# Sparse attention before two expert layers: the first mask and its count as one ScalarE pass, GpSimd's products in another order

## The chip, the cores and the metric

The kernel runs on one core of a Trainium2 chip. The metric is the device time of one launch in microseconds (us). A core has five engines that run their own instruction streams and meet only at semaphores: TensorE (PE in the profile; its weight loads are PEld), VectorE (DVE), ScalarE (ACT), GpSimd (POOL) and SyncE (SP), which here only issues DMAs.

## The reference

Three stages follow one another. Only the first is touched by the change. For each of 32 heads (4 batches by 8 heads) of 576 rows:

```python
scores = scale * np.matmul(q, k.transpose(0, 1, 3, 2))          # 576 x 576 per head
kth = np.partition(scores, -top_k, axis=-1)[..., -top_k:-top_k + 1]   # top_k = 32
mask = scores >= kth
scores = np.where(mask, scores, -1000000000.0)
...
attn = attn / (np.sum(attn, axis=-1, keepdims=True) + 1e-09)
return np.matmul(attn, v)
```

Then the 2304 rows go through a gated layer of 8 experts (each row to one expert, 512 to 1024 to 512) and through a last layer with a softmax-weighted activation and a layer norm.

## The kernel before

`stage_a` does the attention. Two heads make a pair; a pair has NT = 9 tiles of 128 query rows (the ninth holds the last 64 rows of both heads), so there are 16 x 9 = 144 tiles. Everything is float32. Each tile passes through all engines:

- TensorE `scores` (L518) makes the 128 x 576 scores, ScalarE `save_scores` (L306) copies them to SBUF.
- VectorE finds the 24 largest (SURE = 24) from eight chunks of 72: eight MAX8 over the chunks (L425) give 64 candidates, and three MAX8 with two MATCH_REPLACE between them (L453, L458, L461, L464, L470) give the top 24 of those.
- VectorE `work` (L481) marks with 1.0 every score that is below the 24th. GpSimd `rest` (L258) multiplies score by mark, so that what is left is the scores outside the 24. ScalarE `count` (L329) sums the marks, which tells how many scores lie below the 24th.
- VectorE takes the eight largest of the rest (L467), and the pick (L474, a scalar_tensor_tensor of nine elements with a sum) chooses the 32nd value by that count: `thr`.
- VectorE `kept` (L485) marks with 1.0 every score at or over `thr`, and writes over `rests`. GpSimd `mask` (L271) multiplies the exponentials (ScalarE `exp`, L320) by it.
- TensorE turns the result (L526, L527), ScalarE copies it to SBUF (L334, L335), TensorE multiplies by v (L536), ScalarE saves the output (L344).

The order on every engine is written out by hand: one step of VectorE (`quick_step`) handles the last part of tile t, the top 24 of tile t + 1 and the chunks of tile t + 2, interleaved. GpSimd runs rest(t + 1), mask(t), rest(t + 2), mask(t + 1) and so on. The buffers are counted: six for scores (SB), three for probabilities (PB), two for `rests`. A wait is a `wait_ge` on a semaphore; `hold` puts a trivial wait in front of it.

After the 144 tiles `check_quick` takes the minimum of all thresholds. Where a row's count matched none of the nine counts allowed, its `thr` is 0, and a second copy of `stage_a` with the exact method (four MAX8 and three MATCH_REPLACE over all 576 columns) does the whole attention again. In the profiled run it does not.

Of the kernel before, what the change touches and what calls it, by code (L numbers as in the profile page):

```python
# [21 lines left out]
P = 128  # L22
# [21 lines left out]
AHEAD = 4  # L44
RANKED_TOGETHER = (2, 2, 2, 3)
# [16 lines left out]
def at_least(eng, sem, value):  # L62

    if isinstance(value, int) and value <= 0:
        return
    eng.wait_ge(sem, value)

# [10 lines left out]
def build_program(nc, q_t, k_t, v, modality, w_gate, bias, w1, w2, w_in, w_out, g_ln, out):  # L78
    with ExitStack() as ctx:
# [26 lines left out]
        with ExitStack() as ab:  # L106
# [7 lines left out]
            low = sb(ab, "low", [P, PAIRS])  # L114
            again = sb(ab, "again", [1, 1], I32)
            stage_a(nc, q_t, k_t, v, bank, ident, x_all, locals(), True)
            check_quick(nc, bank, ident, low, again)
            stage_a(nc, q_t, k_t, v, bank, ident, x_all, locals(), False)
# [4 lines left out]
def check_quick(nc, bank, ident, low, again):  # L123

    with ExitStack() as ctx:
        row_low = ctx.enter_context(nc.sbuf_tensor("row_low", [P, 1], F32))
        all_low = ctx.enter_context(nc.sbuf_tensor("all_low", [1, 2], F32))
        step, turned = [ctx.enter_context(nc.semaphore(name)) for name in ("check_step", "low_turned")]
        block = ctx.enter_context(nc.Block())

        @block.vector
        def _(dve):
            dve.tensor_reduce(row_low[:, :], low[:, :], AX.X, ALU.min).then_inc(step, 1)
            dve.wait_ge(turned, 1)
            dve.tensor_reduce(all_low[:, 0:1], bank[0][0:1, 0, 0:P], AX.X, ALU.min).then_inc(step, 1)
            dve.wait_ge(step, 2)
            dve.tensor_scalar(all_low[:, 1:2], all_low[:, 0:1], 0.0, None, ALU.is_le).then_inc(step, 1)
            dve.wait_ge(step, 3)
            dve.tensor_copy(again[:, :], all_low[:, 1:2]).then_inc(step, 1)
            dve.wait_ge(step, 4)  # L140

        @block.tensor
        def _(pe):
            pe.wait_ge(step, 1)
            pe.transpose(bank[0][0:1, 0, 0:P], row_low[:, :], ident[:, :]).then_inc(turned, 1)


def stage_a(nc, q_t, k_t, v, bank, ident, x_all, g, quick):
# [3 lines left out]
    const_set = g["const_set"]  # L152
    with ExitStack() as ctx:
        def sem(name):
            return ctx.enter_context(nc.semaphore(name if quick else name + "_again"))

        def sb(name, shape, dt=F32):
            return ctx.enter_context(nc.sbuf_tensor(name if quick else name + "_again", shape, dt))

        def run(eng, program):  # L160

            if quick:
                program()
            else:
                flag = eng.value_load(g["again"][0:1, 0:1], min_val=0, max_val=1)
                with eng.If_ne(eng.to_reg(flag), 0):
                    program()
# [10 lines left out]
        rests = sb("rests", [P, 2, S])  # L178
        unread = sb("unread", [P, S], mybir.dt.bfloat16)
        cand = sb("cand", [P, 2, CAND])  # L180
        below = sb("below", [P, PB])
        pick = sb("pick", [P, TOPK - SURE + 1])
        thr = sb("thr", [P, 2 * NT])
# [9 lines left out]
        max_found = sem("max_found")  # L193
        max_ready = sem("max_ready")
        exped = sem("exped")
        below_ready = sem("below_ready")
        counted = sem("counted")
        rested = sem("rested")
        kept = sem("kept")
        lows = sem("lows")  # L200
# [9 lines left out]
        def _(sp):  # L210
# [11 lines left out]
            def for_later():  # L222

                sp.dma_start(g["mod_sb"][:, :, :], g["modality"]).then_inc(g["route_loaded"], 16)
                sp.dma_start(g["wg_sb"][:, :, :], g["w_gate"].rearrange("(c p) e -> p c e", p=P)).then_inc(g["route_loaded"], 16)
                sp.dma_start(g["wg_heads"][:, :, :], g["w_gate"].rearrange("(h p) e -> p h e", p=DH)).then_inc(g["route_loaded"], 16)
                sp.dma_start(g["bias_sb"][:, :, :].rearrange("p m e -> p (m e)"),
                             g["bias"].rearrange("m e -> (m e)").unsqueeze(0).to_broadcast([P, 2 * E])).then_inc(g["route_loaded"], 16)
                sp.dma_start(g["g_sb"][:, :], g["g_ln"]).then_inc(g["ffn_loaded"], 16)

            def program():
# [7 lines left out]
                if quick:  # L239
                    for_later()  # L240
# [11 lines left out]
        def _(pool):  # L252
            def rest(t, s):

                b = s % PB
                pool.wait_ge(below_ready, t + 1)
                at_least(pool, masked, t - 1)
                pool.tensor_tensor(rests[:, s % 2, :], score[:, s % SB, :], work[:, b, :], ALU.mult).then_inc(rested, 1)  # L258

            def mask(t, s):  # L260
                b = s % PB
                if quick:
                    keeps = rests[:, s % 2, :]
                else:
                    keeps = score[:, s % SB, :]
                    hold(pool, (ranked, t + 1), (exped, t + 1))
                    pool.tensor_scalar(keeps, score[:, s % SB, :], top[:, s % SB, TOPK - 1:TOPK], None,
                                       ALU.is_ge).then_inc(kept, 1)
# [4 lines left out]
            def pair(i, par, more):  # L273
                for j in range(NT):
                    t, s = i * NT + j, par * NT + j
                    if quick and (more or s < 2 * NT - 1):
                        rest(t + 1, (s + 1) % (2 * NT))
                    mask(t, s)

            def program():  # L280
# [3 lines left out]
                if quick:  # L284
                    rest(0, 0)
                (every_pair if quick else all_pairs)(pool, pair)

            if quick:
                pool.memset(x_all[:, :, FULL, :], 0.0).then_inc(const_set, 1)
                pool.memset(ident[:, :], 0.0).then_inc(const_set, 1)  # L290
                pool.wait_ge(const_set, 2)
                pool.affine_select(out=ident[:, :], in_=ident[:, :], compare_op=ALU.not_equal, fill=1.0, base=0,
                                   pattern=[[-1, P]], channel_multiplier=1).then_inc(const_set, 1)

                pool.iota(g["counts"][:, :], pattern=[[1, TOPK - SURE + 1]], base=S - TOPK, channel_multiplier=0,
                          allow_small_or_imprecise_dtypes=True).then_inc(const_set, 1)
                pool.wait_ge(const_set, g["N_CONST"])
# [3 lines left out]
        def _(act):  # L301
# [7 lines left out]
            def negate_max(t, s):  # L309

                j = s % SB
                act.wait_ge(max_found, t + 1)
                act.activation(neg_max[:, j:j + 1], top[:, j, 0:1], ACT.Copy, scale=-SCALE).then_inc(max_ready, 1)

# [7 lines left out]

            def count(t, s):

                b = s % PB
                act.wait_ge(below_ready, t + 1)
                at_least(act, kept, t - PB + 1)
                at_least(act, counted, t)
                act.activation(unread[:, :], work[:, b, :], ACT.Copy, accum_out=below[:, b:b + 1]).then_inc(counted, 1)  # L329
# [21 lines left out]
            def pair(i, par, more):  # L351
                last = par == 1 and not more
                for j in range(NT):
                    t, s = i * NT + j, par * NT + j
                    if quick and (j + 1 < NT or not last):
                        negate_max(t + 1, (s + 1) % (2 * NT))
                    if quick:
                        count(t, s)
# [13 lines left out]
            def program():  # L372
                if quick:
# [1059 lines left out]
```

## Time and profile before

| what | us |
|---|---|
| median of 3 runs (1150.1 to 1154.91) | 1152.74 |
| the profiled execution | 1150.48 |
| its span, from the first to the last instruction | 1148.8 |
| GpSimd's first mask product starts at | 18.36 |
| GpSimd's last but one mask product starts at | 540.54 |
| GpSimd's last mask product starts at | 542.67 |
| the check on the thresholds starts at | 548.49 |

The attention takes 549 us of the 1149. What follows, from 555.7 us on, is routing and the two layers, which the change leaves as they are. In a stage of 144 equal tiles the thing to read is the period: how far one tile's instruction is from the next tile's.

### The profile page before, as it was taken

The page shows a single profiled execution, that of the slowest core. Times are in us where ns is not written, and L with a number is a line of the kernel's source. Part 1 is how long each engine was busy: PE and PEld are TensorE (multiplying, and loading weights), DVE is VectorE, ACT ScalarE, POOL GpSimd, SP SyncE. Part 2 cuts the span into 40 slices and gives each one's busy share as a digit, 9 for nine tenths or more (in the row PEclk, how much of TensorE's full clock was granted, in tenths as well). Part 3 has the DMA queues.
Part 4 walks back from the last instruction along what each step waited for, and adds up shares of the span by engine and source line. Part 5 has one row for each costly group of instructions (what it writes and reads, how often), then busy time and mean ns, then how long its engine had stood idle before and what let it go on. Part 6 is the DMA issues. An engine that isn't in the chain of part 4 may idle for free. (4 is left out here: it accounts for less than half of the span.)

```text
span 1148.8 us, 22766 instructions
## 1 busy us (share of the span) xinstructions
PE 972.8 (85%) x6187; PEld 805.9 (70%) x6187; DVE 795.1 (69%) x3415; ACT 559.3 (49%) x1442; POOL 544.2 (47%) x451
## 2 busy tenths in 40 slices
PE   7888888888887887887664899999999999999985
PEld 4666666666665666666443888898988989888874
DVE  6999999999999999998685352534435254352523
ACT  5888777887777877776221221212212121331211
POOL 4888888888888888887262011111111111441101
PEclk9999999999999999999885999999999999999997
DMA  2001111010111110100623101000000102200000
GB/s 66 28 29 33 33 34 34 12 33 23 34 33 33 34 32 13 31 3 2 232 83 133 52 19 38 10 27 18 18 18 18 37 9 100 91 18 17 21 10 7
DMA packets 38199, 43.66 MB, mean 38 GB/s; under 512 B 24785, under 2 KB 24785, under 8 KB 38098
## 3 DMA queue, kind: packets, MB, share of 16 engines
q1 hardware_dynamic: 34738, 32.06, 8.8%
q0 software_dynamic: 3360, 10.49, 2.8%
q8 instruction: 35, 0.57, 0.2%
q14 instruction: 66, 0.54, 0.2%
HBM read 70.84 MB, written 9.96 MB: 70 GB/s over the span
## 5 line engine op out<-in xcount | busy, mean ns | idle before, releaser
L258 POOL TENSOR_TENSOR rests<-score,work 128x576 f32<-128x576 f32 x144 | 232.7, 1616 | 110.2 <-DVE work L481 110.2
L425 DVE MAX8 cand<-score 128x8 f32<-128x72 f32 x1152 | 214.8, 216 | 9.3 <-ACT score L306 9.1
L536 PE MATMUL bank<-v_sb,prob_t 128*128 128x129 f32 (+1 forms) x1440 | 214.2, 286 | 0.0
L271 POOL TENSOR_TENSOR prob<-prob,rests 128x576 f32<-128x576 f32 x144 | 202.2, 1404 | 0.7 <-DVE rests L485 0.7
L536 PEld LDWEIGHTS bank<-v_sb,prob_t 128*128 128x128 f32 (+1 forms) x1440 | 184.3, 191 | 17.8 <-issue 0.2
L526 PE MATMUL bank<-ident,prob 128*128 128x128 f32 x576 | 95.7, 289 | 103.7 <-POOL prob L271 103.5
L518 PE MATMUL bank<-k_sb,q_sb 64*128 64x288 f32 (+1 forms) x576 | 176.7, 432 | 5.0 <-DMA k_sb<-k_t 4.7
L526 PEld LDWEIGHTS bank<-ident,prob 128*128 128x128 f32 x576 | 61.1, 142 | 168.5 <-POOL prob L271 168.5
L334 ACT ACTIVATE prob_t<-bank 128x512 f32<-128x512 f32 x144 | 86.1, 598 | 108.9 <-PE bank L527 108.8
L518 PEld LDWEIGHTS bank<-k_sb,q_sb 64*128 64x128 f32 (+1 forms) x576 | 100.2, 194 | 26.3 <-issue 6.7
L320 ACT ACTIVATE prob<-score,neg_max 128x576 f32<-128x576 f32 x144 | 110.5, 767 | 0.1
L467 DVE MAX8 top<-rests 128x8 f32<-128x576 f32 x144 | 108.9, 757 | 1.7 <-POOL rests L258 1.6
L1078 POOL TENSOR_SCALAR stat<-stat 128x1 f32<-128x1 f32 x20 | 4.5, 227 | 212.5 <-DVE stat L1233 212.4
L329 ACT ACTIVATE unread<-work 128x576 bf16<-128x576 f32 x144 | 96.9, 673 | 0.0
L306 ACT ACTIVATE score<-bank 128x576 f32<-128x576 f32 x144 | 93.1, 647 | 7.1 <-PE bank L518 6.7
L1310 PE MATMUL bank<-h_t_hi,w_hi 128*128 128x256 f32 x320 | 90.1, 281 | 4.6 <-DVE w_lo L1285 4.6
L1310 PE MATMUL bank<-x_t_hi,w_hi 128*128 128x256 f32 x320 | 91.1, 285 | 1.4 <-DVE x_t_lo L1192 1.4
L1136 ACT ACTIVATE e<-bank,stat 128x1024 f32<-128x1024 f32 x20 | 24.1, 1207 | 136.7 <-DVE stat L1218 136.7
L1310 PE MATMUL bank<-x_t_hi,w_lo 128*128 128x256 f32 x320 | 90.2, 282 | 0.0
L1310 PE MATMUL bank<-h_t_hi,w_lo 128*128 128x256 f32 x320 | 90.1, 281 | 0.0
L1310 PE MATMUL bank<-x_t_lo,w_hi 128*128 128x256 f32 x320 | 90.0, 281 | 0.0
L1310 PE MATMUL bank<-h_t_lo,w_hi 128*128 128x256 f32 x320 | 89.9, 281 | 0.0
(177 smaller groups left out, 2134.3 us busy)
## 6 DMA issues: line engine op xcount, KB each, us to landing
raw<-w SPq DMA_DIRECT2D x22, 2048.0 KB
q_sb<-q_t SPq DMA_DIRECT2D x16, 320.0 KB, 3.0
k_sb<-k_t SPq DMA_DIRECT2D x16, 288.0 KB, 3.2
v_sb<-v SPq DMA_DIRECT2D x32, 128.0 KB, 2.3
x_rows<-x_n SPq DMA_DIRECT2D x16, 256.0 KB
win_sb<-w_in SPq DMA_DIRECT2D x1, 2048.0 KB, 8.2
wout_sb<-w_out SPq DMA_DIRECT2D x1, 2048.0 KB, 13.6
v_sb<-v SPq DMA_DIRECT2D x32, 16.0 KB, 2.1
```

The lines of the kernel that those rows point to most:

```text
L258: pool.tensor_tensor(rests[:, s % 2, :], score[:, s % SB, :], work[:, b, :], ALU.mult).then_inc(rested, 1)
L271: pool.tensor_tensor(prob[:, b, :], prob[:, b, :], keeps, ALU.mult).then_inc(masked, 1)
L306: act.activation(score[:, j, :].rearrange("p (b s) -> p b s", b=2), score_ps[s % 2][:, :, 0:HALF], ACT.Copy).then_inc(saved, 1)
L320: act.activation(prob[:, s % PB, :], score[:, j, :], ACT.Exp, bias=neg_max[:, j:j + 1], scale=SCALE).then_inc(exped, 1)
L329: act.activation(unread[:, :], work[:, b, :], ACT.Copy, accum_out=below[:, b:b + 1]).then_inc(counted, 1)
L334: act.activation(prob_t[:, s % 2, 0:FULL, :], pt_ps[:, 0, :], ACT.Copy)
L425: ins = dve.max(cand[:, s % 2, 8 * c:8 * c + 8], score[:, s % SB, c * CW:(c + 1) * CW])
L467: next_best = mark(dve.max(top[:, s % SB, SURE:TOPK], rests[:, s % 2, :]))
L518: last = pe.matmul(score_ps[s % 2][:, half, 0:HALF], q_sb[par][rows, c * P:(c + 1) * P], k_sb[par][rows, half * HALF:(half + 1) * HALF], s ...
L526: pe.transpose(pt_ps[:, 0, c * P:(c + 1) * P], prob[:, s % PB, c * P:(c + 1) * P], ident[:, :])
L536: last = pe.matmul(out_ps[s % 2], prob_t[0:k, s % 2, c, :], v_sb[par][0:k, c, :], start=(c == 0), stop=(c == KC - 1))
L1310: ins = pe.matmul(dst, lhs[a][:, c, l_at], rhs[b][:, c, r_at], start=(c == 0 and n == 0), stop=(c == chunks - 1 and n == len(parts) - 1))
```

## The change

The diff does these things in the attention (now `attend_quick`; the second, exact copy is `attend_again`):

1. VectorE's `work` pass over 576 columns (L481 before) is gone. In its place VectorE multiplies the 24th value, one number per row, by a constant (`edge`, 128 x 1), and ScalarE computes Sign(edge - score * scale) over the 576 columns: +1 below the 24th value, -1 from it upwards. Its accumulated sum (`balance`) is the number below less the number at or above, so the counts that the pick compares with go in steps of two. The separate `count` pass of ScalarE is gone. GpSimd multiplies score by side: what is at or over the 24th turns negative, what is below stays.
2. The scale is 2^40 (1 - 2^-24) on both sides. VectorE's product is rounded to float32; the 24th value itself counts as at or above if ScalarE's product is not rounded before the subtraction. `check_quick` also looks whether any edge has all mantissa bits set, where this does not hold; six small instructions are in front of its transpose instead of one.
3. GpSimd runs mask(t), rest(t + 2). rest(t + 2) now waits for the pick of tile t + 1 (`picked`).
4. VectorE's step spans four tiles (t, t + 2 and t + 3) and has the pick in its middle. The minimum over a pair's thresholds (L492) is gone.
5. TensorE's order is turn, values, scores (before: scores, turn, values); scores run six tiles ahead. The turned tile has five equal transposes (`prob` is padded with zeros to 640 columns), and ScalarE copies it in one instruction.
6. Most waits are one `wait_ge` instead of `hold`.

The diff, cut to what the text below speaks of:

```diff
@@ check_quick @@
-            dve.tensor_reduce(row_low[:, :], low[:, :], AX.X, ALU.min).then_inc(step, 1)
+            dve.tensor_reduce(row_low[:, :], bounds[:, :, :].rearrange("p b t -> p (b t)"), AX.X, ALU.min).then_inc(step, 1)
+            dve.tensor_scalar(digits[:, :], bounds[:, 1, :].bitcast(I32), MANTISSA, None, ALU.bitwise_and).then_inc(step, 1)
...
+            dve.tensor_scalar(in_range[:, :], row_digits[:, :], float(MANTISSA), None, ALU.is_lt).then_inc(step, 1)
+            dve.wait_ge(step, 5)
+            dve.tensor_tensor(row_fine[:, :], row_low[:, :], in_range[:, :], ALU.mult).then_inc(step, 1)
@@ attend_quick @@
+            def rest(t, s):
+
+
+                pool.wait_ge(sided, t + 1)
+                at_least(pool, masked, t - 1)
+                at_least(pool, picked, t)
+                pool.tensor_tensor(rests[:, s % 2, :], score[:, s % SB, :], side[:, s % 2, :], ALU.mult).then_inc(rested, 1)
...
+            pool.iota(g["counts"][:, :], pattern=[[2, TOPK - SURE + 1]], base=S - 2 * TOPK, channel_multiplier=0,
+                      allow_small_or_imprecise_dtypes=True).then_inc(const_set, 1)
+            pool.wait_ge(const_set, g["N_CONST"])
+            rest(0, 0)
+            rest(1, 1)
+            for t in range(TILES):
+                mask(t, t % WRAP)
+                if t + 2 < TILES:
+                    rest(t + 2, (t + 2) % WRAP)
...
+            def take_sides(t, s):
+
+                act.wait_ge(edge_ready, t + 1)
+                at_least(act, rested, t - 1)
+                at_least(act, picked, t - PB + 1)
+                act.activation(side[:, s % 2, :], score[:, s % SB, :], ACT.Sign, bias=g["edge"][:, t:t + 1],
+                               scale=-EDGE_SCALE, accum_out=balance[:, s % PB:s % PB + 1]).then_inc(sided, 1)
...
+            for t in range(4):
+                save_scores(t, t)
+            for t in range(2):
+                negate_max(t, t)
+                exp(t, t)
+            take_sides(0, 0)
+            save_scores(4, 4)
+            take_sides(1, 1)
+            negate_max(2, 2)
+            for t in range(TILES):
+                if t + 2 < TILES:
+                    take_sides(t + 2, (t + 2) % WRAP)
+                if t + 3 < TILES:
+                    negate_max(t + 3, (t + 3) % WRAP)
+                if t + 2 < TILES:
+                    exp(t + 2, (t + 2) % WRAP)
+                if t >= 2:
+                    save_out(t - 2, (t - 2) % WRAP)
+                if t + 5 < TILES:
+                    save_scores(t + 5, (t + 5) % WRAP)
+                save_turned(t, t % WRAP)
...
+                if rest:
+                    wait_all(dve, (rested, t + 1))
+                    dve.max(top[:, s % SB, SURE:TOPK], rests[:, s % 2, :]).then_inc(rest_found, 1)
...
+                if rest:
+                    wait_all(dve, (rest_found, t + 1), (sided, t + 1))
+                    dve.scalar_tensor_tensor(out=pick[:, :], in0=g["counts"][:, :], scalar=balance[:, s % PB:s % PB + 1],
...
+                if chain:
+                    wait_all(dve, (sure_found, c + 1))
+                    dve.tensor_scalar(g["edge"][:, c:c + 1], top[:, jc, SURE - 1:SURE], EDGE, None, ALU.mult).then_inc(edge_ready, 1)
+                if chunks:
+                    candidates(7).then_inc(cand_done, 1)
+                if rest:
+                    wait_all(dve, (picked, t + 1))
+                    dve.tensor_scalar(rests[:, s % 2, :], score[:, s % SB, :], g["thr"][:, t:t + 1], None, ALU.is_ge).then_inc(kept, 1)
@@ stage_a @@
-                if chain:
-                    hold(dve, (rank_step, sure))
-                    dve.tensor_scalar(work[:, b_next, :], score[:, j, :], top[:, j, SURE - 1:SURE], None,
-                                      ALU.is_lt).then_inc(below_ready, 1)
```

How the order moves on VectorE in the middle of the attention, one step, before (the names are out<-in; `work` is the first mask, `thr` the threshold):

```order
L453 MAX top<-cand 128x8
L425 MAX cand<-score 128x8 x2
L458 MATCH_REPLACE cand<-top,cand 128x64
L425 MAX cand<-score 128x8 x2
L461 MAX top<-cand 128x8
L425 MAX cand<-score 128x8 x2
L464 MATCH_REPLACE cand<-top,cand 128x64
L467 MAX top<-rests 128x8
L470 MAX top<-cand 128x8
L425 MAX cand<-score 128x8
L474 SCALAR_TENSOR_TENSOR pick,thr<-counts,below,top 128x9
L425 MAX cand<-score 128x8
```

Behind it stand L481 and L485, the two passes over 576 columns. And the same step of the change (line numbers are those of the changed kernel; `bounds` holds both thr and edge):

```order
L378 MAX top<-cand 128x8
L373 MAX cand<-score 128x8
L384 MATCH_REPLACE cand<-top,cand 128x64
L373 MAX cand<-score 128x8 x2
L389 MAX top<-rests 128x8
L392 MAX top<-cand 128x8
L395 SCALAR_TENSOR_TENSOR pick,bounds<-counts,balance,top 128x9
L373 MAX cand<-score 128x8
L402 MATCH_REPLACE cand<-top,cand 128x64
L373 MAX cand<-score 128x8 x2
L407 MAX top<-cand 128x8
```

Behind it stand a chunk, the edge (L412, 128x1), the last chunk and the one pass that is left (L417, kept). The pick went from the tenth place to the seventh, and seven instructions and kept now stand behind it.

On GpSimd, in the middle of the attention, before:

```order
L258 TENSOR_TENSOR rests<-score,work 128x576 [waits masked,below_ready]
L271 TENSOR_TENSOR prob<-prob,rests 128x576 [waits exped,kept]
L258 TENSOR_TENSOR rests<-score,work 128x576 [waits masked,below_ready]
L271 TENSOR_TENSOR prob<-prob,rests 128x576 [waits exped,kept]
L258 TENSOR_TENSOR rests<-score,work 128x576 [waits masked,below_ready]
```

And in the change:

```order
L266 TENSOR_TENSOR rests<-score,side 128x576 [waits picked,masked,sided]
L271 TENSOR_TENSOR prob<-prob,rests 128x576 [waits exped,kept]
L266 TENSOR_TENSOR rests<-score,side 128x576 [waits picked,masked,sided]
L271 TENSOR_TENSOR prob<-prob,rests 128x576 [waits exped,kept]
L266 TENSOR_TENSOR rests<-score,side 128x576 [waits picked,masked,sided]
```

The two products still alternate. Before, the rest product waits for VectorE's first mask and the mask product behind it finds its operands ready. Now both wait for VectorE in every tile: mask for kept, rest for the pick of the next tile.

## Rows read from the trace of the kernel before

**Rows 1.** The page, its first line: the span.

```profile
span 1148.8 us, 22766 instructions
```

**Rows 2.** Windows: length; busy of PE, PEld, DVE, ACT, POOL; clock, DMA, GB/s.

```profile
18.36:540.54 522.18, 421.92 (x2672) 323.06 (x2672) 517.16 (x2838) 412.32 (x1145) 423.65 (x286) 1.00 0.09 26
```

**Rows 3.** Timeline of VectorE: start, length, engine, line, operation, tiles, idle before.

```profile
402.81 0.51 DVE L485 TENSOR_SCALAR rests<-score,thr 128x576 f32<-128x576 f32 x1
403.24 0.21 DVE L453 MAX8 top<-cand 128x8 f32<-128x64 f32 x1
403.37 0.35 DVE L425 MAX8 cand<-score 128x8 f32<-128x72 f32 x2
403.64 0.07 DVE L458 MATCH_VALUE_LOAD cand<-top,cand 128x8 f32 x1
...
403.83 0.35 DVE L425 MAX8 cand<-score 128x8 f32<-128x72 f32 x2
...
404.69 0.76 DVE L467 MAX8 top<-rests 128x8 f32<-128x576 f32 x1
405.36 0.21 DVE L470 MAX8 top<-cand 128x8 f32<-128x64 f32 x1
...
405.62 0.36 DVE L474 SCALAR_TENSOR_TENSOR pick<-counts,below,top 128x9 f32<-128x9 f32 x1
405.91 0.08 DVE L474 DVE_READ_ACCUMULATOR pick<-counts,below,top 128x1 f32 x1
...
406.06 0.50 DVE L481 TENSOR_SCALAR work<-score,top 128x576 f32<-128x576 f32 x1
```

**Rows 4.** Timeline of GpSimd: first products, one period, last products.

```profile
13.13 1.40 POOL L258 TENSOR_TENSOR rests<-score,work 128x576 f32<-128x576 f32 x1 [9.46 <-DVE work L481]
...
18.36 1.40 POOL L271 TENSOR_TENSOR prob<-prob,rests 128x576 f32<-128x576 f32 x1
...
402.96 1.62 POOL L258 TENSOR_TENSOR rests<-score,work 128x576 f32<-128x576 f32 x1 [0.68 <-DVE work L481]
404.55 1.40 POOL L271 TENSOR_TENSOR prob<-prob,rests 128x576 f32<-128x576 f32 x1
406.63 1.62 POOL L258 TENSOR_TENSOR rests<-score,work 128x576 f32<-128x576 f32 x1 [0.68 <-DVE work L481]
...
540.54 1.40 POOL L271 TENSOR_TENSOR prob<-prob,rests 128x576 f32<-128x576 f32 x1
542.67 1.40 POOL L271 TENSOR_TENSOR prob<-prob,rests 128x576 f32<-128x576 f32 x1 [0.74 <-DVE rests L485]
```

**Rows 5.** Timeline of VectorE: the first pick, and the last kept.

```profile
15.86 0.23 DVE L474 SCALAR_TENSOR_TENSOR pick<-counts,below,top 128x9 f32<-128x9 f32 x1 [0.20 <-ACT unread L329]
16.01 0.09 DVE L474 DVE_READ_ACCUMULATOR pick<-counts,below,top 128x1 f32 x1
...
542.07 0.52 DVE L485 TENSOR_SCALAR rests<-score,thr 128x576 f32<-128x576 f32 x1
```

**Rows 6.** Line L781 (least, median, most ns), timeline of GpSimd, of VectorE.

```profile
L781 DVE TENSOR_SCALAR wout_sb<-wout_sb,g_sb x8: 473/474/9082, 576.0 to 587.4; 128x512 f32<-128x512 f32 x8
...
576.22 9.02 POOL L950 TENSOR_TENSOR win_lo<-win_sb,win_hi 128x4096 fp32r<-128x4096 f32 x1 [10.37 <-DVE win_hi L779]
...
576.44 9.08 DVE L781 TENSOR_SCALAR wout_sb<-wout_sb,g_sb 128x512 f32<-128x512 f32 x1
```

**Rows 7.** Timeline of GpSimd and VectorE: a 128x1 operation beside a long product.

```profile
1011.25 9.06 POOL L1063 TENSOR_TENSOR w_lo<-raw,w_hi 128x4096 fp32r<-128x4096 f32 x1 [11.92 <-ACT w_hi L1110]
...
1016.15 0.14 DVE L1224 TENSOR_SCALAR stat<-stat 128x1 f32<-128x1 f32 x1
```

**Rows 8.** Timeline of ScalarE: the start of the attention, the first count pass.

```profile
13.36 0.65 ACT L306 ACTIVATE score<-bank 128x576 f32<-128x576 f32 x1 [1.27 <-PE bank L518]
...
14.96 0.67 ACT L329 ACTIVATE unread<-work 128x576 bf16<-128x576 f32 x1
15.54 0.19 ACT L329 ACTIVATION_READ_ACCUMULATOR unread<-work 128x1 f32 x1
```

More of the change, by code:

```diff
@@ L44 @@
 AHEAD = 4
+EDGE_SCALE = 2.0**40 * (1.0 - 2.0**-24)
+EDGE = 2.0**40 * (1.0 - 2.0**-24)
+LEAST = 2.0**-60
+MANTISSA = 2**23 - 1
+TILES = PAIRS * NT
+UNITS = [(2 * c, 2 * c + 1) for c in range(FULL)] + [(2 * FULL,)]
 RANKED_TOGETHER = (2, 2, 2, 3)
@@ L66, in at_least, with wait_all @@
     eng.wait_ge(sem, value)
+def wait_all(eng, *counts):
+    for sem, n in counts:
+        eng.wait_ge(sem, n)
 def hold(eng, *counts):
@@ L137, in _ @@
-            dve.tensor_scalar(all_low[:, 1:2], all_low[:, 0:1], 0.0, None, ALU.is_le).then_inc(step, 1)
-            dve.wait_ge(step, 3)
+            dve.wait_ge(step, 7)
+            dve.tensor_scalar(all_low[:, 1:2], all_low[:, 0:1], LEAST, None, ALU.is_le).then_inc(step, 1)
+            dve.wait_ge(step, 8)
             dve.tensor_copy(again[:, :], all_low[:, 1:2]).then_inc(step, 1)
-            dve.wait_ge(step, 4)
+            dve.wait_ge(step, 9)
         @block.tensor
         def _(pe):
-            pe.wait_ge(step, 1)
@@ L252, in _ @@
         def _(pool):
[L253 to L258, printed above, removed]
             def mask(t, s):
                 b = s % PB
[L262 to L268, printed above, removed]
+                keeps = score[:, s % SB, :]
+                hold(pool, (ranked, t + 1), (exped, t + 1))
+                pool.tensor_scalar(keeps, score[:, s % SB, :], top[:, s % SB, TOPK - 1:TOPK], None,
+                                   ALU.is_ge).then_inc(kept, 1)
                 pool.wait_ge(kept, t + 1)
@@ L275, in pair @@
                     t, s = i * NT + j, par * NT + j
-                    if quick and (more or s < 2 * NT - 1):
-                        rest(t + 1, (s + 1) % (2 * NT))
                     mask(t, s)
@@ L283, in program @@
                 pool.wait_ge(ones_set, 2)
[L284 to L297, printed above, removed]
+                all_pairs(pool, pair)
             run(pool, program)
@@ L321, in exp @@
                                bias=neg_max[:, j:j + 1], scale=SCALE).then_inc(exped, 1)
[L323 to L329, printed above, removed]
             def save_turned(t, s):
@@ L354, in pair @@
                     t, s = i * NT + j, par * NT + j
[L355 to L358, printed above, removed]
                     if j + 1 < NT or not last:
@@ L372, in program @@
             def program():
-                if quick:
-                    act.wait_ge(const_set, g["N_CONST"])
                 for j in range(AHEAD):
                     save_scores(j, j)
-                if quick:
-                    negate_max(0, 0)
                 exp(0, 0)
-                (every_pair if quick else all_pairs)(act, pair)
+                all_pairs(act, pair)
             run(act, program)
@@ L487, in quick_pair @@
-            def quick_pair(i, par, more):
-                at_least(dve, lows, i - 1)
-                for j in range(NT):
-                    left = 2 * NT if more else 2 * NT - (par * NT + j)
-                    quick_step(i * NT + j, par * NT + j, chain=left > 1, more=left > 2)
-                dve.tensor_reduce(g["low"][:, bass.ds(i, 1)], thr[:, par * NT:(par + 1) * NT], AX.X, ALU.min).then_inc(lows, 1)
-            def program():
-                if quick:
-                    dve.wait_ge(const_set, g["N_CONST"])
-                    quick_step(-1, -1, first=True)
-                    every_pair(dve, quick_pair)
-                    dve.wait_ge(lows, PAIRS)
-                else:
-                    all_pairs(dve, ranked_pair)
+            def program():
+                all_pairs(dve, ranked_pair)
@@ L556, in program @@
                     scores(j, j, 0)
-                (every_pair if quick else all_pairs)(pe, pair)
+                all_pairs(pe, pair)
             run(pe, program)
@@ L564, in is_first @@
     return isinstance(t, int) and t < n
-def every_pair(eng, pair):
-    for i in range(PAIRS):
-        pair(i, i % 2, i < PAIRS - 2)
 def all_pairs(eng, pair):
```

321 lines of the change are left out of this document (229 added, 92 removed).

## The prediction, made before the changed kernel ran

> **What bounds the kernel now.** I read the views in this order: the windows by stage, then the timelines of VectorE and GpSimd over one tile, then the durations of single instructions where something else runs beside them.
>
> The profiled execution took 1150.48 us, with a span of 1148.8 [rows 1]. The changed part is the attention. From the first mask product at 18.36 us to the last but one at 540.54 are 142 periods [rows 4], so 522.18 / 142 = 3.68 us on average; in the undisturbed middle a rest product starts at 402.96 and the next at 406.63, a period of 3.67. In that stretch VectorE is busy for 517 of 522 us, GpSimd 424, TensorE 422, ScalarE 412 [rows 2]. VectorE looks like the bound, with no idle time. The timeline says more. The first pick, at 15.86, runs while GpSimd stands still: its accumulator is read 0.15 us after it starts. In the middle the pick starts at 405.62 and the read comes 0.29 later, at 405.91 [rows 3, 5]. What it waits for is on GpSimd: the mask product ran from 404.55 for 1.40, to 405.95 [rows 4]. So VectorE seems busy for 0.14 us of each tile in which the pick only stands behind GpSimd's product. VectorE's own work is 3.67 - 0.14 = 3.53.
>
> This makes the bound a loop over two engines. VectorE's first mask starts (402.39, 3.67 before the row at 406.06), the rest product starts 0.57 later, the mask product 1.59 behind it (404.55), the pick is let go 1.36 later (405.91), the next first mask starts 0.15 later: 0.57 + 1.59 + 1.36 + 0.15 = 3.67. That is the whole period.
>
> Two more things must be read, since both of GpSimd's products share something with VectorE. The rest product takes 1.62 where `kept` runs beside its beginning, and 1.40 at 13.13, before any `kept` was there [rows 4]. And the other way round, with the same kind of instruction as `kept` (tensor_scalar, float32, SBUF to SBUF): L781 takes 474 ns in the usual case of its eight, and the one that started at 576.44, when a GpSimd product had been running from 576.22, took 9082 ns. It ended at 585.52, the product at 585.24 [rows 6]. So whichever of the two begins first has the way, and the other stands still: a held tensor_scalar ends 0.28 us after the product that held it.
>
> **The change part by part.** I follow a new period from the start of mask(t), called M. VectorE's `kept` ended 0.08 before it (542.07 + 0.52 to 542.67, [rows 4, 5]) and its next instruction starts 0.08 before an end of `kept` (402.81 + 0.51 against 403.24 [rows 3]), so at M - 0.16.
>
> From there to the pick: MAX8 of the candidates 0.13, one chunk 0.14, match 0.19 (403.64 to 403.83), two chunks 0.27, MAX8 over the rest 0.67 (404.69 to 405.36), MAX8 0.13 [rows 3]. Sum 1.53, so the pick would start at M + 1.37. Two of these now stand nearer to what they need than before: the match is one chunk behind its MAX8, and the pick is 0.80 behind the start of a MAX8 that takes 0.76. Waits can add 0 to 0.10 in all; no row shows them at such a distance, and I take 0.03: M + 1.40. GpSimd's mask product ends at M + 1.40 and is out of the way just then, so the pick is not held: 0.15 to its read, 0.09 for the read [rows 5], 0.08 for GpSimd to see it. Rest(t + 2) starts at M + 1.72. No `kept` runs beside it now, so I take 1.40 and not 1.62: it ends at M + 3.12.
>
> Meanwhile VectorE goes on from the read of the pick at M + 1.55: a chunk 0.15, match 0.19, two chunks 0.27, MAX8 0.13, chunk 0.14, edge, chunk 0.14. The edge is a 128 x 1 operation that the attention did not have before; the nearest row is L1224 with 0.14 in all [rows 7], and as a step to the next 0.08 to 0.14. Sum 1.10 to 1.16, so `kept` is reached at M + 2.65 to 2.71. This is 0.4 before rest(t + 2) ends. By [rows 6] it is held and ends 0.28 + 0.04 (576 columns, not 512) behind it, at M + 3.44, and mask(t + 1) starts at M + 3.52.
>
> **The new period is 3.52**, 0.15 less than 3.67. The ends: no waits at all, 3.49, and a few hundredths of rounding under it, 3.46; waits of 0.10, 3.59. VectorE alone would need 0.43 + 1.53 + 0.03 + 0.15 + 1.10 = 3.24: the pass taken away (0.42 us a tile: its 0.50 less the 0.08 by which the next one starts ahead of its end) and the pick's 0.14 are nearly all gained on VectorE, and GpSimd's chain of two waits takes back two thirds of that.
>
> The Trainium skill states this on the page "SBUF — State Buffer", section "Who interferes with whom": VectorE in a two-port mode and GpSimd take a shared pair of ports as a lock, the one that issues first has it for the whole instruction and the other "fully blocks". The trace agrees, with 9082 ns against 474 in rows 6.
>
> Other engines. ScalarE loses a count pass and one of two copies and gets the sign pass, which I cost as the count pass: 0.67, and its sum at 0.77 [rows 8]. Busy 412 / 142 = 2.90 a tile before [rows 2], so it fits in 3.52. Its deadline: the edge of t + 2 is ready about M - 0.7, the side then at M + 0.3 even if it stands behind a copy, and rest(t + 2) asks for it at M + 1.72. More than a microsecond is left. If that cover went, each tenth would count 14 us. TensorE: 422 / 142 = 2.97 a tile, cover 0.5. The turned tile of t leaves TensorE before the next mask product ends either way; the new order of TensorE and its run six tiles ahead I cost at nothing, hidden in that half microsecond; with the cover gone (period under 3.0) TensorE would be next. The two DMA waits of SyncE only change their place by tiles that are far apart.
>
> The start. Before, mask(0) starts at 18.36. Now ScalarE does four score copies, exp(0) and exp(1) before the first sign pass. The fourth copy starts at 13.36 and ends at 14.01, two small ones and two exps follow (0.67 each as steps, 0.3 for the small ones), so the sign pass starts at 15.65 and its sum is there at 16.42. Rest(0) 16.50 to 17.90, MAX8 over it from 18.00, the pick at 18.86, read at 19.10, rest(1) 19.18 to 20.58, `kept` held to 20.90, mask(0) at 20.98: +2.6.
>
> The end. From the last mask product to the check nothing changes. The last interval, 2.13, has no rest product in it before or after and stays at 2.1. The check gets five more small VectorE instructions and a reduce over 288 numbers instead of 16: 5 x 0.14 (the size of L1224 [rows 7]) to 0.21, and 0.3, with their waits 1.2 us. The sixteen small reduces L492 are inside the old average.
>
> **Sum.** Mask(142) starts at 20.98 + 142 x 3.52 = 520.8, where it was 540.54: -19.7. The check gives +1.2: -18.5. The profiled execution would be 1150.48 - 18.5 = 1132.0. The median of the runs shown is 1152.74, 2.3 above the profiled one, so in its terms 1134.2.
>
> **Rivals.**
>
> *The edge is held too (slower).* If the 128 x 1 edge takes the same way as `kept`, VectorE comes to it at M + 2.43, while the rest product runs, and stands until that is over, at about M + 2.93 (0.19 before its recorded end, as L781's 9082 - 474 ns imply); then edge, chunk and a whole `kept` follow one after the other behind it: 0.08 + 0.14 + 0.51 + 0.08 and the edge's own start, M + 3.75. 142 x 0.23 = 33 more, 1167 us. It decides from a hold of about 0.1 on. Against it: L1224, a 128 x 1 tensor_scalar, took 0.14 at 1016.15 with a GpSimd product running from 1011.25 to 1020.31 [rows 7]. I give it 6 in 100. The same section of the Trainium skill names tensor_scalar among the operations that can take the pair and exempts no size; by that rule alone the edge would be held and this rival would be the forecast. Row 1016.15 speaks against that reading.
>
> *The rest product takes 1.62 whatever runs beside it (slower).* Then 3.74 a period, 142 x 0.22 = 31 more, 1165 us. For it: all steady ones take 1.62. Against it: the one at 13.13 takes 1.40. 4 in 100.
>
> *The redo runs.* If ScalarE rounds the product before it subtracts, the 24th value gives 0 and not -1, no count matches, and the exact copy runs: 144 tiles x 7 passes x 0.67 = 675 us more, about 1810. Nothing in the trace shows such a pass. 2 in 100. The Trainium skill, page "ScalarE: Activation LUTs", section "Step-by-step: what each stage is for", says that scale and bias are one fused multiply-add with a single rounding; no row here shows it.
>
> *`kept` is not held.* If the pass can run beside the rest product, VectorE is the bound with 3.24: 142 x 0.28 = 40 less, 1094 us. Rows 6 are against it. 7 in 100.
>
> *The gain is eaten by waits.* A period of 3.62 to 3.70, from semaphore waits that I take as 0.03 and that add up over the four engines: 1148 to 1160. For it: the new loop crosses between the engines four times, the old one twice. 13 in 100.
>
> **How the numbers follow.** Forecast with its own bounds (3.46 to 3.59, 1126 to 1144): 64 in 100. What is left, 4 in 100, lies under 1126 without `kept` being free. A measurement of this kernel can tell about 0.5%, 5.8 us. Faster: 64 + 7 + 4 = 75 and 2 of the fifth rival's 13, 77. Same: the rest of it, 11. Slower: 6 + 4 + 2 = 12. The range must leave out at most 2 in 10: I take 1120 to 1158, which leaves out the slower ones (12) and the free `kept` (7).
>
> **What would show it.** In the changed kernel's trace: `kept` with a mean near 0.8 us and not 0.51, its end 0.3 us behind a rest product's end; the pick at 0.23, not 0.36; both GpSimd products at 1.40; GpSimd's idle time divided into 0.3 before rest (released by the pick) and 0.4 before mask (released by `kept`); 3.52 from mask to mask. I am wrong if `kept` takes 0.51 with a product beside it, if the edge takes more than 0.2, if the rest product's wait ends on ScalarE's `side`, or if ScalarE or TensorE show no idle time.

## The result, and the profile after

The changed kernel takes 1137.8 us (median of 4 runs, 1136.92 to 1138.4), against 1152.43 for the kernel before (4 runs). The ratio is 0.9872, with a 95% interval of 0.985 to 0.9894: faster by 14.6 us, or 1.3%, with the slowest of its runs 11.7 us under the fastest of the kernel before. The times here and below are medians of the usual executions; one of the six of e3 took 4580.92 us at a granted clock of 0.202 and is left out. The profiled execution took 1136.92 us, where that of before took 1150.48. It is the forecast case, inside its own bounds (1126 to 1144), 3.6 us over the predicted 1134.2.

One tile on GpSimd in the changed kernel, as in [rows 4] (start, length, engine, line, operation, tiles, and in brackets the idle time before with what ended it):

```profile
20.65 1.40 POOL L271 TENSOR_TENSOR prob<-prob,rests 128x576 f32<-128x576 f32 x1 [0.39 <-DVE rests L417]
...
401.82 1.41 POOL L271 TENSOR_TENSOR prob<-prob,rests 128x576 f32<-128x576 f32 x1 [0.40 <-DVE rests L417]
403.58 1.41 POOL L266 TENSOR_TENSOR rests<-score,side 128x576 f32<-128x576 f32 x1 [0.35 <-DVE pick L395]
405.39 1.41 POOL L271 TENSOR_TENSOR prob<-prob,rests 128x576 f32<-128x576 f32 x1 [0.40 <-DVE rests L417]
...
526.07 1.39 POOL L271 TENSOR_TENSOR prob<-prob,rests 128x576 f32<-128x576 f32 x1
```

Both products take 1.41, where the rest product took 1.62. But GpSimd stops twice per tile now, 0.35 us for the pick and 0.40 for kept; before it stopped once, for 0.68. The period is 405.39 - 401.82 = 3.57, and over all 142 it is (526.07 - 20.65) / 142 = 3.56, where it was 3.68.

One thing said ahead of the prediction must be set right, since the argument leans on it. The products themselves stand in the same order in both kernels: rest(0), rest(1), mask(0), rest(2), mask(1) and so on. What is new on GpSimd is only what they wait for, above all the pick of tile t + 1 ahead of rest(t + 2).

The same stretch on VectorE, the rows that answer to [rows 3]:

```profile
403.18 0.22 DVE L395 SCALAR_TENSOR_TENSOR pick<-counts,balance,top 128x9 f32<-128x9 f32 x1
403.33 0.08 DVE L395 DVE_READ_ACCUMULATOR pick<-counts,balance,top 128x1 f32 x1
...
404.20 0.14 DVE L412 TENSOR_SCALAR bounds<-top 128x1 f32<-128x1 f32 x1
404.25 0.23 DVE L373 MAX8 cand<-score 128x8 f32<-128x72 f32 x1
404.40 0.91 DVE L417 TENSOR_SCALAR rests<-score,bounds 128x576 f32<-128x576 f32 x1
405.23 0.21 DVE L378 MAX8 top<-cand 128x8 f32<-128x64 f32 x1
```

The pick is free, 0.22 us instead of 0.36. (Counted in the two orders shown ahead of the prediction, it went from the fourteenth instruction of the step to the eighth, with eight instructions and `kept` behind it; the tenth, seventh and seven given there are miscounted.) The edge runs in the middle of a rest product and takes 0.14. `kept` starts at 404.40 and takes 0.91, where it took 0.51 before, and ends at 405.31, which is 0.32 after the rest product ends (403.58 + 1.41 = 404.99). VectorE shows no idle time at all. Its busy time hides 0.4 us of standing per tile.

The window from the first to the last but one mask product, as [rows 2] (length; busy of PE, PEld, DVE, ACT, POOL; clock):

```profile
20.65:526.07 505.42, 420.48 (x2671) 322.23 (x2672) 504.02 (x2816) 418.80 (x1001) 399.57 (x284) 1.00 0.10 27
```

### The profile page after: what moved, and what is told of

The parts are those of the page before. It is cut to its first block and busy times, and to the rows that moved or that the text cites. A ratio compares the mean times of both kernels' runs of the same rounds, so it can differ in the third digit from the quotient of the medians.

```text
span 1135.2 us, 21099 instructions
## 1 busy us (share of the span) xinstructions
PE 971.1 (86%) x6187; PEld 805.2 (71%) x6187; DVE 783.7 (69%) x3404; ACT 566.6 (50%) x1298; POOL 519.8 (46%) x452
## 5 line engine op out<-in xcount | busy, mean ns | idle before, releaser
L373 DVE MAX8 cand<-score 128x8 f32<-128x72 f32 x1152 | 227.8, 223 | 8.3 <-ACT score L297 8.3
L266 POOL TENSOR_TENSOR rests<-score,side 128x576 f32<-128x576 f32 x144 | 203.0, 1410 | 63.7 <-DVE pick L395 51.2
L445 PE MATMUL bank<-ident,prob 128*128 128x128 f32 x720 | 111.3, 286 | 90.8 <-POOL prob L271 90.8
L445 PEld LDWEIGHTS bank<-ident,prob 128*128 128x128 f32 x720 | 77.0, 142 | 155.1 <-POOL prob L271 154.6
L322 ACT ACTIVATE prob_t<-bank 128x640 f32<-128x640 f32 x144 | 101.2, 703 | 85.1 <-PE bank L445 85.0
L417 DVE TENSOR_SCALAR rests<-score,bounds 128x576 f32<-128x576 f32 x144 | 130.6, 907 | 0.1
L305 ACT ACTIVATE side<-score,bounds 128x576 f32<-128x576 f32 x144 | 110.4, 766 | 2.2 <-DVE bounds L412 2.2
```

The lines of the kernel that those rows point to most:

```text
L305: act.activation(side[:, s % 2, :], score[:, s % SB, :], ACT.Sign, bias=g["edge"][:, t:t + 1], scale=-EDGE_SCALE, accum_out=balance[:, s % ...
L322: act.activation(prob_t[:, s % 2, :, :].rearrange("p c q -> p (c q)"), turned_ps[:, 0:QW], ACT.Copy).then_inc(turned_sb, 1)
L373: ins = dve.max(cand[:, sa % 2, 8 * n:8 * n + 8], score[:, sa % SB, n * CW:(n + 1) * CW])
L417: dve.tensor_scalar(rests[:, s % 2, :], score[:, s % SB, :], g["thr"][:, t:t + 1], None, ALU.is_ge).then_inc(kept, 1)
L445: ins = pe.transpose(turned_ps[:, c * P:(c + 1) * P], prob[:, s % PB, c * P:(c + 1) * P], ident[:, :])
```

## The experiments

The theory is the prediction's: the period is a loop, mask product, pick, rest product, held `kept`, mask product. All experiments start from the changed kernel (1137.8 us). "The period" is always the distance between two mask products, and its mean over 142 tiles is read from the start of the first to the start of the last but one. The rivals are VectorE's total work, TensorE's order, and that `kept` is slow by itself. No run takes single parts out of the change, so how the 0.12 us a tile that it gained divide between the removed pass, the moved pick and the shorter waits is not shown.

### Without the wait for the pick

```diff
             def rest(t, s):
...
                 at_least(pool, masked, t - 1)
-                at_least(pool, picked, t)
```

> Edit: the changed kernel, but rest(t + 2) on GpSimd no longer waits for the pick of tile t + 1. Theory (the period is the loop mask, pick, rest, kept, with the pick just reaching VectorE 0.04 us before the mask product ends and so getting in ahead of the rest product): GpSimd's 0.35 us of idle time before rest falls to about 0.05, the rest product ends 0.29 us earlier, the held kept with it, period 3.57 to about 3.28, 142 tiles x 0.29 = 40 us less, 1097. Rival (the wait is what protects the pick: without it the rest product begins first and holds the pick for its whole length): pick of 1.5 us, period near 4.4, about 1260. Rival (VectorE's own work or TensorE is the bound): 1138.

Measured: 1110.55 us, 27.3 less. GpSimd and VectorE:

```profile
403.43 1.41 POOL L270 TENSOR_TENSOR prob<-prob,rests 128x576 f32<-128x576 f32 x1 [0.40 <-DVE rests L416]
404.98 1.41 POOL L265 TENSOR_TENSOR rests<-score,side 128x576 f32<-128x576 f32 x1
406.79 1.41 POOL L270 TENSOR_TENSOR prob<-prob,rests 128x576 f32<-128x576 f32 x1 [0.39 <-DVE rests L416]
...
404.80 0.22 DVE L394 SCALAR_TENSOR_TENSOR pick<-counts,balance,top 128x9 f32<-128x9 f32 x1
...
406.01 0.70 DVE L416 TENSOR_SCALAR rests<-score,bounds 128x576 f32<-128x576 f32 x1
```

The pick, at 404.80, still gets in before the rest product at 404.98. `kept` is reached at the same distance from the mask product as before (2.58 us) and is held 0.2 us less, since the rest product ends 0.21 earlier. So the wait for the pick cost 3.56 - 3.36 = 0.20 us a tile, not the 0.29 that I had put down: the rest product also waits for the mask product's own semaphore, and behind that it starts 0.14 after the mask product's end (403.43 + 1.41 to 404.98) and not 0.05. VectorE's instructions were not touched, and neither of the two rivals, 1260 and 1138, fits.

### The pick earlier, and later

In e2 two chunks move from ahead of the pick to behind it, in e3 one moves the other way. VectorE executes the same instructions in all three.

```diff
@@ e2 @@
-                if chunks:
-                    candidates(1, 2)
                 if rest:
                     wait_all(dve, (rested, t + 1))
...
                 if chunks:
-                    candidates(3)
+                    candidates(1, 2, 3)
@@ e3 @@
+                if chunks:
+                    candidates(3)
                 if rest:
                     wait_all(dve, (rest_found, t + 1), (sided, t + 1))
...
-                if chunks:
-                    candidates(3)
```

> Edit: the changed kernel, with the two chunk MAX8 that stand ahead of the MAX8 over the rest moved behind the pick. VectorE's work is the same, only the pick comes 0.27 us earlier. Theory: the pick is then held by the mask product until that ends, its read comes 0.05 us before the end (0.16 us earlier than now), so the period goes from 3.57 to 3.41, 142 x 0.16 = 22 us less, 1115, and pick takes 0.35 us again. Rival (VectorE's total work sets the period): 1138 or more, since the hold of the pick is added.

> Edit: the changed kernel, with one chunk MAX8 that stands behind the pick moved ahead of it, so the pick comes 0.13 us later. VectorE's work is the same. Theory (loop through the pick): rest starts 0.13 later, period 3.57 to 3.70, 142 x 0.13 = 19 us more, 1157. Rival (VectorE's total work sets the period, the order does not matter): 1138.

Measured: 1118.64 us for the early pick (19.2 less), 1156.17 for the late one (18.4 more). GpSimd in e2, then in e3:

```profile
403.38 1.40 POOL L271 TENSOR_TENSOR prob<-prob,rests 128x576 f32<-128x576 f32 x1 [0.40 <-DVE rests L415]
404.98 1.41 POOL L266 TENSOR_TENSOR rests<-score,side 128x576 f32<-128x576 f32 x1 [0.20 <-DVE pick L393]
406.79 1.40 POOL L271 TENSOR_TENSOR prob<-prob,rests 128x576 f32<-128x576 f32 x1 [0.40 <-DVE rests L415]
```

```profile
404.23 1.40 POOL L271 TENSOR_TENSOR prob<-prob,rests 128x576 f32<-128x576 f32 x1 [0.40 <-DVE rests L417]
406.12 1.41 POOL L266 TENSOR_TENSOR rests<-score,side 128x576 f32<-128x576 f32 x1 [0.48 <-DVE pick L397]
407.92 1.40 POOL L271 TENSOR_TENSOR prob<-prob,rests 128x576 f32<-128x576 f32 x1 [0.40 <-DVE rests L417]
```

Only the bracket before the rest product moves: 0.20, 0.35, 0.48. The periods are 3.41 and 3.69 (3.42 and 3.68 as means). In e2 the pick takes 0.34 again, because it is now there before the mask product ends. One chunk of 0.13 us more in front of the pick costs 18.4 us, more than the whole gain of the change, with the same instructions on VectorE: its total work is not the bound.

### Is `kept` held, or slow by itself?

```diff
-                    dve.tensor_scalar(rests[:, s % 2, :], score[:, s % SB, :], g["thr"][:, t:t + 1], None, ALU.is_ge).then_inc(kept, 1)
+                    dve.tensor_scalar(rests[:, s % 2, :], score[:, s % SB, :], g["thr"][:, t:t + 1], 0.0, ALU.is_ge, ALU.add,
+                                      accum_out=n_kept[:, :]).then_inc(kept, 1)
```

> Edit: the changed kernel, with kept also writing out a sum that nobody reads, which makes it another form of tensor_scalar. Theory (kept takes 0.91 us because the rest product holds it, and this form is not held): it takes 0.6 to 0.75 us beside the running product, with 0.08 for the sum, mask starts 3.45 to 3.55 us after the mask before, 1121 to 1135. Rival (kept takes 0.91 for another reason, or every form is held): 0.91 and more, plus the read of the sum, period 3.65, 1149 or more.

Measured: 1123.79 us, 14.0 less. Two rows of GpSimd and two of VectorE from the middle, then the last `kept` of the attention and the mask product behind it:

```profile
403.19 1.42 POOL L267 TENSOR_TENSOR rests<-score,side 128x576 f32<-128x576 f32 x1 [0.36 <-DVE pick L396]
404.89 1.41 POOL L272 TENSOR_TENSOR prob<-prob,rests 128x576 f32<-128x576 f32 x1 [0.28 <-DVE rests L418]
...
404.00 0.80 DVE L418 TENSOR_SCALAR_CACHE_REDUCE rests<-score,bounds 128x576 f32<-128x576 f32 x1
404.73 0.08 DVE L418 DVE_READ_ACCUMULATOR rests<-score,bounds 128x1 f32 x1
...
512.69 0.81 DVE L418 TENSOR_SCALAR_CACHE_REDUCE rests<-score,bounds 128x576 f32<-128x576 f32 x1
...
513.59 1.41 POOL L272 TENSOR_TENSOR prob<-prob,rests 128x576 f32<-128x576 f32 x1 [0.97 <-DVE rests L418]
```

This form is slower alone, 0.81 us at 512.69 while GpSimd stands idle for 0.97, against some 0.50 for the plain form. But it is not held: in the middle it takes 0.80, from 404.00 to 404.80, while the rest product runs to 404.61, and the mask product starts at 404.89. (I had expected 0.6 to 0.75.) In the changed kernel `kept` ended 0.32 after the rest product, here 0.19, and could be earlier if it were reached earlier. That the slower instruction gives the faster kernel shows that the 0.91 us are a hold. The period, 3.45, is now VectorE's own chain: VectorE has no idle time and none of its instructions is held.

The Trainium skill says the same on the page "SBUF — State Buffer", section "Who interferes with whom": the form of tensor_scalar that also writes out its accumulator is excepted from those that can take the shared pair. The trace agrees, with 0.80 us beside a product and 0.81 without one, against 0.91 for the plain form held.

### TensorE's order

The diff puts TensorE's order of before (scores five tiles ahead, first in the step) back; the five equal transposes and the single copy stay.

```diff
-            for t in range(6):
+            for t in range(5):
                 scores(t, t)
             for t in range(TILES):
+                if t + 5 < TILES:
+                    scores(t + 5, (t + 5) % WRAP)
                 turn(t, t % WRAP)
                 if t >= 1:
                     values(t - 1, (t - 1) % WRAP)
-                if t + 6 < TILES:
-                    scores(t + 6, (t + 6) % WRAP)
```

> Edit: the changed kernel, with TensorE's order of before (scores first, five tiles ahead; then turn, values). Theory: TensorE has over 0.5 us of idle time in each period and is not in the loop: 1138, within 3 us. Rival (part of the gain is TensorE's new order): some of the 14.6 us are lost, 1141 to 1152.

Measured: 1138.47 us, period 3.56. The new order of TensorE is worth nothing that can be measured here, and it costs nothing.

### Who asks first

With e1's edit the rest product still waits for the mask product's own semaphore. Three buffers for `rests` instead of two take this wait away.

```diff
-        rests = sb("rests", [P, 2, S])
+        rests = sb("rests", [P, 3, S])
...
-                at_least(pool, masked, t - 1)
-                at_least(pool, picked, t)
+                at_least(pool, masked, t - 2)
```

(and `s % 3` for `s % 2` where `rests` is used.)

> Edit: as e1_no_pick_wait, with three buffers for rests, so the rest product waits for an older mask product and can follow the one before it at once. Theory (the loop is now GpSimd's alone: 1.41 + 0.14 + 1.41 + 0.40 = 3.36): if the pick, which comes 0.04 us before the mask product ends, still gets in first, the 0.14 goes down to 0 or 0.05, period 3.22 to 3.27, 1110 less 13 to 20 = 1090 to 1098. If the rest product now gets in first, the pick is held for the whole product (1.5 us instead of 0.22), period about 4.4, near 1260. The trace says which; VectorE's own work (3.2) allows no less than about 3.22.

Measured: 1251.02 us, 113 more. The trace says which, GpSimd first, then VectorE:

```profile
400.67 1.40 POOL L270 TENSOR_TENSOR prob<-prob,rests 128x576 f32<-128x576 f32 x1 [1.60 <-DVE rests L416]
402.03 1.41 POOL L265 TENSOR_TENSOR rests<-score,side 128x576 f32<-128x576 f32 x1
405.03 1.40 POOL L270 TENSOR_TENSOR prob<-prob,rests 128x576 f32<-128x576 f32 x1 [1.60 <-DVE rests L416]
...
402.03 1.43 DVE L394 SCALAR_TENSOR_TENSOR pick<-counts,balance,top 128x9 f32<-128x9 f32 x1
...
404.45 0.50 DVE L416 TENSOR_SCALAR rests<-score,bounds 128x576 f32<-128x576 f32 x1
```

Both start at 402.03, and the rest product wins. An operation on nine elements stands for 1.43 us (the median of its 144; only at the two ends of the attention is it shorter), and the period is 4.36 here and 4.35 in the mean. TensorE's granted clock is lower in this run, 0.87 between 100 and 500 us where the changed kernel has 1.00, but GpSimd waits for nothing but `kept` in that stretch, and VectorE has no idle time, so this is not what makes the period long. So the changed kernel's wait for the pick does have a purpose when nothing else separates the two products; it is only dearer than needed.

> Edit: as e5_three_rests, with the pick 0.27 us earlier as in e2_pick_early, so it is queued well before the mask product ends. If the one that asks first has the way: the pick is let in at the mask product's end (0.34 us long), the rest product right behind, period 3.25 to 3.35 (VectorE has 0.12 of hold on top of 3.22), 1092 to 1106. If two products of GpSimd back to back keep VectorE out: pick of 1.7 us or more, period about 4.4, near 1260.

This adds e2's diff to e5's. Measured: 1098.56 us. The two products follow each other as closely as in e5, but the pick is ready before:

```profile
401.06 1.42 POOL L270 TENSOR_TENSOR prob<-prob,rests 128x576 f32<-128x576 f32 x1 [0.50 <-DVE rests L414]
402.42 1.43 POOL L265 TENSOR_TENSOR rests<-score,side 128x576 f32<-128x576 f32 x1
...
402.15 0.35 DVE L392 SCALAR_TENSOR_TENSOR pick<-counts,balance,top 128x9 f32<-128x9 f32 x1
```

The same pick is let in when it comes 0.27 us earlier: 1251 against 1099 us, from the place of two MAX8. So it is not that two products back to back keep VectorE out. `kept` takes 0.49 us and is not held any more; VectorE is the bound, with 3.28, of which 0.13 are the pick standing behind the mask product.

> Edit: the changed kernel with both e1's edit (no wait for the pick) and e2's (pick earlier). Theory: the rest product waits for the mask product's own semaphore, 0.14 us, in which the queued pick gets in; VectorE is not the bound, so it is the same as e1_no_pick_wait: period 3.36, 1110. Rival (each of the two edits has its own gain and they add): 1110 - 19 = 1091.

Measured: 1108.87 us, period 3.36, the same as e1 (3.36) within 2 us. The gains of e1 and e2 do not add, since both shorten the same gap before the rest product, down to 0.14.

> Edit: as e6_early_three_rests, with one of the two chunk MAX8 put back ahead of the pick. Theory: what decides is who asks first. The pick is then ready 1.22 us after the mask product starts, the rest product asks at 1.36, so the pick still gets in, and it no longer stands 0.13 us behind the mask product. VectorE's period 3.27 goes to about 3.15; GpSimd's own 1.36 + 1.42 + 0.40 = 3.18 takes over: 3.18 to 3.22, 1098.6 less 7 to 13, 1086 to 1092. Rival (0.14 us is too near and the rest product gets in first): pick of 1.5 us, near 1250, or some tiles so and others not, between.

The diff against e6: `candidates(1)` ahead of the MAX8 over the rest, `candidates(2, 3)` behind the pick. Measured: 1084.83 us, a ratio to the kernel before of 0.9416 (0.9395 to 0.9437). The pick takes 0.22, and the period is 3.18:

```profile
402.65 1.41 POOL L270 TENSOR_TENSOR prob<-prob,rests 128x576 f32<-128x576 f32 x1 [0.40 <-DVE rests L416]
404.02 1.42 POOL L265 TENSOR_TENSOR rests<-score,side 128x576 f32<-128x576 f32 x1
405.83 1.41 POOL L270 TENSOR_TENSOR prob<-prob,rests 128x576 f32<-128x576 f32 x1 [0.39 <-DVE rests L416]
...
403.88 0.22 DVE L394 SCALAR_TENSOR_TENSOR pick<-counts,balance,top 128x9 f32<-128x9 f32 x1
```

The pick starts 1.23 us after the mask product, 0.14 ahead of the rest product, and this is enough throughout (median 0.22 over all 144 picks, mean period 3.18). The time is 1.2 us under the lower end of what I had expected.

### The first sign passes ahead of the first exponentials

```diff
-            for t in range(2):
-                negate_max(t, t)
-                exp(t, t)
             take_sides(0, 0)
-            save_scores(4, 4)
             take_sides(1, 1)
+            save_scores(4, 4)
+            for t in range(2):
+                negate_max(t, t)
+                exp(t, t)
             negate_max(2, 2)
```

> Edit: as e9_pick_between, and at the start of the attention ScalarE does the first two sign passes before the first two exponentials. Theory: the first rest product starts about 1.8 us earlier (the first sign pass at 13.4 instead of 15.2), the period is untouched: e9 less 1 to 2 us, at the edge of what can be told. Rival: exp(0) is now late for mask(0) and eats it, no change.

Measured: 1083.11 us, 1.7 less than e9 (a ratio of 0.9393, 0.9373 to 0.9414; the two intervals overlap, though the slowest run of the four, 1083.53, is under the fastest of e9, 1084.80). In its trace the first mask product starts at 19.04, where it started at 20.81 in e9, 1.8 us earlier. It is the fastest version of the study, 54.7 us under the changed kernel.

The mean periods beside the times: 3.18 gives 1084.8, 3.28 gives 1098.6, 3.36 gives 1110.6, 3.42 gives 1118.6, 3.45 gives 1123.8, 3.56 gives 1137.8, 3.68 gives 1156.2, 4.35 gives 1251.0. From one to the next 142 times the difference of the periods answers to the difference of the times within 3 us, so what these versions differ by is the period and nothing beside it.

## Why the prediction was right, point by point

**The reading of the kernel before**, a loop of GpSimd and VectorE with holds in it, gave the right forecast, but no experiment was made on that kernel, and 3.53 of its 3.67 us are VectorE's own work by the prediction's count. What e2 and e3 show is the loop in the changed kernel, by moving the time both ways with the same instructions.

**The period** was put at 3.52 and is 3.56. The terms, from the mask product at 401.82:

| term | forecast | measured |
|---|---|---|
| mask product to the start of the pick | 1.40 | 1.36 |
| pick to its read, and the read | 0.24 | 0.23 |
| end of the read to the rest product | 0.08 | 0.17 |
| rest product | 1.40 | 1.41 |
| end of it to the end of `kept` | 0.32 | 0.32 |
| to the next mask product | 0.08 | 0.08 |

The term that was mis-sized is the one from the read of the pick to the rest product. I took the 0.08 that GpSimd needs behind a finished pass; behind the pick it is 0.17. That the pick ends with the read of an accumulator does not explain it: in e4 `kept` ends with such a read too, at 404.81, and the mask product starts 0.08 later. The rest product stands behind three waits, the pick's last, and the mask product behind two, `kept`'s first; whether that makes the difference was not tried. The 0.03 us that I had added for waits on VectorE were not there (1.37 with none, 1.36 measured). The two misses go opposite ways, so the sum is nearer than its terms: 0.04 us a tile, 142 x 0.04 = 5.7 us. The 3.6 us between the medians flatter the forecast a little. Between the profiled executions it is 4.9 (1136.92 against 1132.0).

**The hold of `kept`** was the step that turned some 60 us taken off VectorE (an estimate of the prediction) into a gain of 15, and it came out to the hundredth (0.28 + 0.04 forecast, 0.32 measured). I expected the instruction near 0.8 us; it is 0.91 since VectorE comes to it at 2.58 after the mask product, not at 2.65 to 2.71. That changed nothing, as the end is set by GpSimd. e4 shows that it is a hold.

**The start** was put 2.6 us later, and is 2.3 later (20.65 against 18.36). **The check** was put at +1.2: from its first instruction to the next stage it is 8.31 us (533.96 to 542.27) against 7.23 (548.49 to 555.72), +1.1. Sum in the profiled executions: start +2.29, 142 periods 505.42 - 522.18 = -16.76, last interval -0.07, check +1.1, together -13.4; their spans differ by 13.6.

**The rivals.** The held edge fell: 0.14 us in the middle of a product in every tile. The rest product at 1.62 whatever runs beside it fell: 1.41. The redo did not run, since with it some 675 us would have been added; that ScalarE's product is not rounded before the subtraction is therefore what the counts imply, though no experiment was made for it. The free `kept` fell. Waits adding up did happen in one place, with 0.09, just under the 0.10 to 0.18 a tile that this rival needed; in all the period came out 0.04 longer. ScalarE's sign pass takes 0.77 where I had costed it as the count pass with 0.67; it lay under its cover, with 0.66 us of idle time in ScalarE's period.

## What to carry to other kernels

Busy time on VectorE can be standing time, 0.41 us of each tile here: compare one instruction's length where GpSimd is idle with its length beside a GpSimd product before you believe that VectorE is the bound. Where two engines hold each other up, the gain of a pass taken away is not its length but what the loop between them loses; write the loop down with its starts and ends. And in such a loop the place of one small instruction can be worth more than the whole change: 0.13 us later it cost 18.4 us, where the change had gained 14.6. A different place for the pick, one wait less and a third buffer for `rests`, with no pass removed, took the kernel from 1137.8 to 1084.8 us.

## What the runs showed of the hardware that I had not expected

- When the pick and a GpSimd product following another without a wait start at the same 0.01 us, the product goes first, in all of the middle of e5 (1.43 us for nine elements). With 0.14 us of lead (e9) the pick goes first there in every tile. What decides nearer than that was not tried.
- GpSimd starts the rest product 0.17 us after the pick's accumulator is read, and the mask product 0.08 after the end of `kept`, with an accumulator (e4) or without. What makes the two differ was not tried. Behind a wait on its own last product it starts 0.14 after that product's end, without the wait 0.04 before it (402.03 against 400.67 + 1.40).
- ScalarE's sign pass with a sum and a float32 output takes 0.77 us, the copy with a sum and a bfloat16 output took 0.67 ([rows 8]) over the same 576 columns. Which of the function, the output type and the bias does it was not tried. The exponential, with float32 output and, like the sign pass, one bias per row, takes 0.76 too (at 402.02 in the changed kernel).
